# The order of work around the third and fourth chunk in the first group of an attention and expert kernel

## The reference

```python
for t in range(S):                                   # attention, one head
    cur = (u * k[t])[:, None] * v[t][None, :]
    y[t] = r[t] @ (state + cur)
    state = w[:, None] * state + k[t][:, None] * v[t][None, :]
xn = (x - mean) / sqrt(var + 1e-6) * g_ln            # x: 1536 rows of 384
x2 = x + relu(xn @ w_ch1) @ w_ch2                    # 384 -> 1536 -> 384
e  = argmax(x2 @ w_gate), or the expert of the row before where the local gate is >= 0.5
out = softmax(x2 @ w_gate)[e] * (relu(x2 @ w1[e]) @ w2[e])   # 8 experts, 384 -> 1024 -> 384
```

## Time and profile before

| what | value |
|---|---|
| runs | 394.37, 392.72, 392.60 us, median 392.72 us |
| profiled execution | 397.39 us |
| its span in the trace | 395.6 us |
| outside the span | 1.8 us |
| PE busy | 381.9 us (97%) |
| VectorE, ScalarE, GpSimd busy | 226.5 us (57%), 161.5 us (41%), 131.0 us (33%) |
| chain that ended last, by engine | PE 89%, POOL 3%, DMA 2%, issue 1%, ACT 1% |

### The profile page before, as it was taken

One profiled execution on the slowest core, in us unless ns is written; L12 is line 12 of the kernel. 1 busy time (PEld: TensorE's weight loads), 2 busy tenths in 40 slices (PEclk: granted clock), 3 DMA queues, 4 the chain that ended last, 5 costly groups with the idle time before them and its releaser, 6 DMA issues.

```text
span 395.6 us, 9033 instructions
## 1 busy us (share of the span) xinstructions
PE 381.9 (97%) x3191; PEld 348.1 (88%) x3191; DVE 226.5 (57%) x468; ACT 161.5 (41%) x299; POOL 131.0 (33%) x114
## 2 busy tenths in 40 slices
PE   8897999999999999999999999999999999999992
PEld 6797999999999999999999845689999999999982
DVE  7897545522633552364567848698566665537440
ACT  5554323322312341232243246287625752555520
POOL 2979680740470163000000302602332233223231
PEclk9996999999999999999999999999999999999997
DMA  7994311500331150500107396599892469111111
GB/s 215 336 330 142 108 41 49 154 35 20 107 106 40 52 152 28 174 8 2 41 2 282 100 315 202 161 372 321 290 362 74 161 204 340 43 32 41 28 43 44
DMA packets 32634, 54.91 MB, mean 139 GB/s; under 512 B 3261, under 2 KB 20323, under 8 KB 32592
## 3 DMA queue, kind: packets, MB, share of 16 engines
q1 hardware_dynamic: 30288, 48.07, 37.1%
q0 software_dynamic: 2304, 6.30, 5.3%
HBM read 49.64 MB, written 5.51 MB: 139 GB/s over the span
## 4 chain that ended last, share of the span: by engine, by line
PE 89%; POOL 3%; DMA 2%; issue 1%; ACT 1%; DVE 0%; SPq 0%; POOLq 0%; DVEq 0%
PE bank L1027 19%; PE bank L927 6%; PE bank L929 6%; PE bank L928 6%; PE bank L1358 5%; PE bank L1330 5%; PE bank L1366 5%; PE bank L1362 5%; PE bank L1334 5%; PE bank L1337 5%; PE bank L1347 3%; PE bank L942 3%; PE bank L1259 3%; PE bank L1236 3%; PE bank L971 2%; DMA arena<-in_v_rows 2%
## 5 line engine op out<-in xcount | busy, mean ns | idle before, releaser
L1027 PE MATMUL bank<-xnT_hi,parts 128*128 128x256 f32 x432 | 67.5, 293 | 1.1 <-issue 0.9
L1027 PEld LDWEIGHTS bank<-xnT_hi,parts 128*128 128x128 f32 x432 | 57.5, 194 | 1.8 <-ACT xnT_hi L709 0.5
L650 POOL DMA_INDIRECT out_y<-late x14 | 20.5, 1462 | 94.0 <-DVE late L1910 94.0
L1553 DVE SCALAR_TENSOR_TENSOR parts<-bank,parts 128x512 fp32r<-128x512 f32 x36 | 24.9, 690 | 43.4 <-ACT parts L716 43.0
L927 PE MATMUL bank<-parts 128*128 128x384 f32 x144 | 49.1, 341 | 0.0
L929 PE MATMUL bank<-parts 128*128 128x384 f32 x144 | 48.2, 335 | 0.0
L928 PE MATMUL bank<-parts 128*128 128x384 f32 x144 | 48.2, 334 | 0.0
L803 ACT ACTIVATE parts<-stage (+1 forms) x32 | 46.2, 1484 | 2.5 <-DMA stage<-in_w 2.2
L716 ACT ACTIVATE parts<-bank 128x512 fp32r<-128x512 f32 x36 | 21.5, 597 | 56.8 <-PE bank L1027 56.2
L1879 DVE TENSOR_TENSOR parts<-stage,parts x24 | 41.1, 1755 | 5.5 <-ACT parts L803 4.8
L1027 PE MATMUL bank<-xnT_lo,parts 128*128 128x256 f32 x216 | 38.0, 286 | 0.0
(11 more groups left out here) (255 smaller groups left out, 736.4 us busy)
## 6 DMA issues: line engine op xcount, KB each, us to landing
stage<-in_w SPq DMA_DIRECT2D x36, 768.0 KB, 6.5
stage<-in_w_ch SPq DMA_DIRECT2D x6, 768.0 KB, 8.5
arena<-in_k_t SPq DMA_DIRECT2D x12, 224.0 KB, 3.7
arena<-in_r_t SPq DMA_DIRECT2D x12, 224.0 KB, 3.0
arena<-in_v_rows SPq DMA_DIRECT2D x12, 192.0 KB, 4.2
arena<-in_k_rows SPq DMA_DIRECT2D x12, 192.0 KB, 3.4
x_rows<-stage SPq DMA_DIRECT2D x12, 192.0 KB, 1.9
arena<-in_r_rows SPq DMA_DIRECT2D x10, 192.0 KB, 3.1
```

The costliest lines, as they stand in the source:

```text
L650: pool.indirect_dma_start(out, bass.IndirectOffsetOnAxis(give[:, s:s + 1], 0), yo[s % 2], None, bounds_check=T - 1, oob_is_err=False).then ...
L1027: mm = pe.matmul(acc, w[:, k, at], x[:, k, :], start=start and k == 0, stop=stop and k == KD - 1, skip_group_check=first and q == 0)
L1553: dve.scalar_tensor_tensor(hT_lo[:, at, :].rearrange("p a t -> p (a t)"), bk[6 + q % 2][:], 0.0, hT_hi[:, at, :].rearrange("p a t -> p (a ...
```

## The change

In the first group alone, four streams are written in another order, and one load gets a semaphore of its own.

- TensorE: scores(3) move from behind pair 3 to behind pair 4 (the fifth), and chunk(3) from behind pair 4 to behind pair 5 (the sixth). The order becomes pair 3, pair 4, scores(3), pair 5, chunk(3), `rows_out(0, 0)`.
- SyncE: `load_rows` issues the k rows first, then r, then v, for every chunk. For chunk 2 the k rows count on the new semaphore `s_k2`. The waits on `s_rows[0]` are 16 lower for all even chunks, since that load no longer counts there.
- GpSimd: `ends(2)` waits for `s_k2` alone. `rows(2)` waits for both semaphores. `rows(3)` moves ahead of `rest_of_piece(4)`.
- TensorE: `gain(2)` waits for `s_rows[0]` too, since it reads the v rows and its other wait no longer implies them.
- VectorE: behind `hidden(0, 3)` the order was masked(3), the sum of chunk 2, its statistics, `rest_of_piece(3)`. It becomes `rest_of_piece(3)`, the sum of chunk 2 (`sums`), masked(3), the statistics (`moments`).

```diff
@@ sync
             def load_rows(c, u):
                 for q in (coef_ready, kend_ready, gain_mm, cv_ready, y_mm):
                     sp.wait_ge(q, c - 1)
+                sp.dma_start(kr[u], k_rows[bass.ds(c * P, P), :]).then_inc(
+                    s_k2 if isinstance(c, int) and c == 2 else s_rows[u], 16)
                 sp.dma_start(rr[u], r_rows[bass.ds(c * P, P), :]).then_inc(s_rows[u], 16)
-                sp.dma_start(kr[u], k_rows[bass.ds(c * P, P), :]).then_inc(s_rows[u], 16)
                 sp.dma_start(vr[u], v_rows[bass.ds(c * P, P), :]).then_inc(s_rows[u], 16)
@@ gpsimd, rows(c)
-                pool.wait_ge(s_rows[u], R_FIRST + R_LOADS * (c // 2))
+                pool.wait_ge(s_rows[u], R_FIRST[u] + R_LOADS * (c // 2))
+                if c == 2:
+                    pool.wait_ge(s_k2, 16)
@@ gpsimd, ends(c)
+                elif c == 2:
+                    pool.wait_ge(s_k2, 16)
                 else:
-                    pool.wait_ge(s_rows[u], R_FIRST + R_LOADS * (c // 2))
+                    pool.wait_ge(s_rows[u], R_FIRST[u] + R_LOADS * (c // 2))
+                if c >= 2:
                     pool.wait_ge(gain_mm, c - 1)
@@ gpsimd, the written-out order
             diagonal(2)
+            rows(3)
             rest_of_piece(4)
-            rows(3)
             diagonal(3)
@@ tensor, gain(c)
                 pe.wait_ge(kend_ready, c + 1)
+                if isinstance(c, int) and c == 2:
+                    pe.wait_ge(s_rows[0], R_FIRST[0] + R_LOADS)
@@ tensor, group(g)
                 if first:
-                    hidden(g, range(3, 4))
+                    hidden(g, range(3, 5))
                     scores(g * 2 + 3, 1, bk[0:2])
+                    hidden(g, range(5, NHP))
+                    chunk(g * 2 + 3, 1, n_lg, ends)
@@ vector, first_group
                 hidden(0, range(3, 4))
+                rest_of_piece(3)
+                sums(2, 0, bk[4])
                 masked(3, bk[0:2], scT[0])
-                rows_of(2, 0, bk[4])
-                rest_of_piece(3)
+                moments(2, 0)
                 hidden(0, range(4, 5))
```

More of the change, by code:

```diff
@@ L278, in build_program @@
         s_pair, s_k1, s_hi0, s_wc = sem("s_pair"), sem("s_k1"), sem("s_hi0"), sem("s_wc")
-        s_mean0 = sem("s_mean0")
+        s_mean0, s_k2 = sem("s_mean0"), sem("s_k2")
         s_v = [sem(f"s_v{u}") for u in range(2)]
@@ L316, in build_program @@
         block = ctx.enter_context(nc.Block())
-        T_LOADS, R_LOADS, R_FIRST = 2 * 16, 3 * 16, 16
+        T_LOADS, R_LOADS, R_FIRST = 2 * 16, 3 * 16, (0, 16)
         T_FIRST = (2 * 16, 16)
@@ L540, in ends @@
                 if c < 2:
-                    pool.wait_ge(s_rows[u], R_FIRST)
+                    pool.wait_ge(s_rows[u], 16)
                     pool.wait_ge(s_endS, 1)
-                else:
-                    pool.wait_ge(s_rows[u], R_FIRST + R_LOADS * (c // 2))
+                elif c == 2:
+                    pool.wait_ge(s_k2, 16)
+                else:
+                    pool.wait_ge(s_rows[u], R_FIRST[u] + R_LOADS * (c // 2))
+                if c >= 2:
                     pool.wait_ge(gain_mm, c - 1)
@@ L1474, in new_state, with sums @@
                                       ALU.add).then_inc(state_ready, 1)
-            def rows_of(c, u, bank):
+            def sums(c, u, bank):
                 dve.wait_ge(y_mm, c + 1)
@@ L1479, in rows_of, with moments @@
                 dve.tensor_tensor(tile_of(c), bank[:, 0:DM], cv[u], ALU.add).then_inc(x_ready, 1)
+            def rows_of(c, u, bank):
+                sums(c, u, bank)
+                moments(c, u)
+            def moments(c, u):
                 dve.wait_ge(x_ready, c + 1)
```

## The result

| | kernel before | changed kernel |
|---|---|---|
| median of 20 executions each, same chip | 394.25 us | 391.79 us |
| lowest and highest | 392.60 and 396.95 us | 390.46 and 392.82 us |
| profiled execution, its span | 397.39 us, 395.6 us | 391.53 us, 389.7 us |

The ratio is 0.9934, with a 95% interval from 0.9917 to 0.9951. The gain is 2.5 us (0.7%), where 5.45 us was forecast, and 391.79 us lies above the range of 386.7 to 390.9 us. Yet the two profiled executions lie 5.9 us apart. The three runs of before that the forecast started from were also on the low side: their median was 392.72 us, that of 20 is 394.25 us. So of the 4.5 us between the forecast of 387.3 us and the measured time, 1.5 us come from where it started and 3.0 us from a gain that was too large.

A forecast was written before the change was run, and what follows sets the result against it. TensorE was taken as the bound. Idle time 2.2 us plus full-clock gains of 0.99, 1.99 and 0.27 us made 5.45 us, so 392.72 - 5.45 = 387.3 us, range 386.7 to 390.9 us.

The forecast's parts named there:

- The bound and the place: TensorE, busy 97% of the span, is the bound; the loss sits in the slice from 30 to 40 us.
- The idle time: TensorE's wait ahead of scores(3) for GpSimd's `decays(3)`, line 525, would go: 2.2 us gained.
- The slow clock: TensorE's half clock from 32.28 to 39.11 us, after the idle stretch, would not occur: 3.25 us gained.
- The three clock terms: Gains at full clock on TensorE: scores 0.99 us, a pair 1.99 us, a gain 0.27 us.
- Rival A: Timed runs lack the slow clock stretch, so only the idle 2.2 us is gained: 390.5 us, chance 0.2.
- Whether the others keep up: Walk of GpSimd and VectorE in the first group: inputs ready when the earlier TensorE wants them, costing nothing.
- the three due times: `rest_of_piece(4)`, `rest_of_piece(5)` and centred rows for `turn_xn(1)`, wanted around `rows_out(0, 0)`: costed at nothing, at most 0.7 us.
- Rival B: GpSimd gains nothing as k lands no earlier; gain 4.2 us, 388.5 us; chance 0.17 with similar smaller slips.
- Rival C: `rest_of_piece(4)` becomes the new long wait in `rows_out` at step 4, clock falls: slower, 393.5 us, chance 0.05.
- Rival D: The gain is given back later, some wait in group 1 absorbing 4 us or more: 392 us, chance 0.08.

The follow-up runs named there:

- e5: The kernel before, unaltered, one more execution with a profile: 394.57 us.
- e6: The kernel before, unaltered, profiled once more for a third draw: 395.92 us.
- e1: The kernel before with 18 small matmuls filling TensorE's wait for `decays(3)`: median 393.80 us, ratio 0.9979.
- e4: The changed kernel unaltered, run again in the first batch of experiments beside the kernel before: median 392.03 us, ratio 0.9953.
- e7: The kernel before with two unneeded products on GpSimd ahead of `decays(3)`, lengthening TensorE's idle stretch: median 396.35 us, ratio 1.0077.
- e2: The kernel before with TensorE's new order alone: median 393.67 us, ratio 0.9992.
- e3: The changed kernel with TensorE's old order: median 392.73 us, ratio 0.9961.
- e10: The changed kernel with VectorE's old order (masked(3), sum and statistics of chunk 2, then `rest_of_piece(3)`): median 394.04 us, ratio 1.0014.
- e8: The changed kernel, but `ends(2)` waits for the r and v rows again as well as k: median 393.25 us, ratio 0.9980.
- e11: The changed kernel with new_state(1) ahead of masked(2) on VectorE, a try for a better version: median 391.88 us, ratio 0.9948.

## Why the prediction was wrong

**The bound and the place: right.** TensorE bounded the kernel there, and the wait for line 525 and the half clock both went from the trace.

**The idle time: right in size for the traced execution, too large at the median.** It was 2.2 us there, 2.4 and 2.1 us in e5 and e6, and would be about 0.9 us where v landed early (e1, from GpSimd's end of `decays(3)`). The executions of before without a fallen clock lie 1.5 us above the changed kernel at the median.

**The slow clock: the step that failed.** The prediction took "the gain over whole", 392.72 - 5.45, and called it an assumption "that the median contains the same slow stretch". It does not. The three clock terms, 3.25 us together, can be in an execution fully only where the granted clock is below 0.990, as in 6 of 83 executions, and about half in 12 more. These shares are estimates from the mean clocks and the times of the groups (2.8 and 1.8 us above the large one). At the median the clock's part comes to 0.3 to 0.5 us, since without those 18 executions it is 393.6 instead of 393.9 us, and 393.4 instead of 393.8 us in the batch of e4. E1 took the fall away and left the median where it was. Next to this, the start from a median of three runs put the forecast another 1.5 us too low. The same profile held the warning: it was 4.7 us above the median it was to explain, and the forecast gave that case a chance of 0.2.

**Rival A: it happened.** Its gain of 2.2 us stands beside the measured 2.5 us (1.8 us in the batch of e4). That the number fits so well is partly luck: it is made of less idle time and a little of the clock. Its mechanism, the clock that falls in some executions only, is shown by e5, e6 and e1. What it lacked is that the idle stretch itself differs between executions with the landing of v. The rule it named from the Trainium skill, "TensorE: Matmul & The Clock Gate", Part 1: The HAM clock gate, that the gate's beat is not tied to the kernel's start, fits the three different outcomes behind four nearly equal idle stretches (2.2, 2.4, 2.1 and, in e7, 2.1 us). No run here shows the beat itself. Its 390.5 us was too low because it started from a median of three runs; 394.25 - 2.2 would have been 392.0 us.

**Whether the others keep up: right, but for the landing of k.** The steps of GpSimd and VectorE in the walk end within 0.3 us of the trace, also for the undone parts: 1.2 us for 1.3 (e2), 0.5 us for 0.3 to 0.5 (e3), 1.3 us for 1.6 (e10). The centring in e2 is an exception. The other is k. The walk let it land between 19.6 and 20.3 us, and in the seven traces with k issued first it landed at 20.4 (e8), 20.8, 21.0, 21.3, 21.3, 21.9 and 23.0 us (e11). Issued second, it had landed at 20.2 to 20.6 us in all six traces with the old order. So GpSimd gains because `ends(2)` no longer waits for v; that the new order of the loads helps is not shown, and the own semaphore with the old order, which may be better, was not tried. Zero for the three due times holds for the changed kernel's own trace. E11 shows that it fails by 0.7 us when k lands late.

**Rival B** did not occur as a whole. Its price, 1.2 us, is what e8 lies above e4, though e8's trace does not show how. **Rival C** did not occur; its wait shows with 0.7 us in one execution of e11. **Rival D** did not occur: the two spans differ by 5.9 us, of which 5.35 us are there at the end of the first group, and nothing was lost later.

**What stays open.** Why v lands at 22.1 us in one execution and at 23.4 us in another was not tried, nor why k lands no earlier when it is issued first. The share of late landings was not counted in untraced executions. So how the 2.5 us divide between idle time and clock rests on the estimate above, and why the gain is 2.5 us in the first comparison and 1.8 us in the batch of e4 is not known. The stop of 0.6 to 1.15 us in pair 0 that some traces show has no explanation either.

## What to carry to other kernels

Before a profile's terms are subtracted from a median, see whether the profiled execution is a typical one: this one was 4.7 us longer than the median and had the lowest granted clock of all, and the terms that made it longer could not be gained in most of the others. A short wait on a transfer costs more than its trace shows or less, since in these runs both its length and what the clock does behind it differed from one execution to the next. So the steadiness of a chain is a gain of its own (the spread of the executions fell from a standard deviation of 1.3 us to 0.6 us). When steps are moved on one engine, walk the due times of all the others: here TensorE's move alone, and everything without VectorE's reordering, were worth nothing measurable, everything without TensorE's move 1.1 us, and all together 1.8 to 2.5 us.

## What the runs showed of the hardware

- An idle stretch of TensorE of 2.1 to 2.4 us had three outcomes in three traces of one program: no fall of the clock (e5), 1.2 GHz for some 3.4 us (e6), and 1.2 GHz for 6.8 us (before). A stretch of 2.1 us in e7 brought no fall either. In the two traces with a fall it came within 0.3 us of the moment when work began again (before: work at 32.32 us, fall at 32.28 us; e6: work at 32.13 us, 0.97 of the clock up to 32.4 us).
- With the stretch 1.3 us longer (e7), 4 of 8 executions had a mean clock below 0.990, against none of 19 beside them.
- The same load, at the same place in the queue, lands at different times: v rows, issued third at 16.2 to 17.3 us, let `ends(2)` start at 22.0, 22.1, 22.3, 23.2, 23.4 and 23.4 us in the six traces with the old order. The issue time does not decide it: issued at 16.15 us they took 7.2 us (before), issued at 17.14 us 4.8 us (e7).
- K rows issued first landed no earlier than issued second: at 20.4 to 23.0 us in seven traces, against 20.2 to 20.6 us in six.
- Where a GpSimd and a VectorE instruction with two inputs in SBUF met in the first group, the later one took longer by the rest of the other: GpSimd's first product of `decays(3)` took 2.82 us in after, where VectorE's subtraction was ahead of it, and 1.27 us in before. A hand-made walk that lets whole instructions take turns gave the starts and ends of GpSimd quoted above to within 0.1 us.
